# Two attention units side by side ahead of the first FFN tile, weight splits beside the FFN tiles, and the last column two feeds earlier

## What is computed

```python
f = 1.0 / (1.0 + np.exp(-f_logit))
for t in range(S):
    state = f[:, :, t, :, None] * state + np.einsum('bhd,bhe->bhde', k[:, :, t], v[:, :, t])
    y[:, :, t] = np.einsum('bhd,bhde->bhe', q[:, :, t], state)
# x = y by token
h = x @ w_in;  x = where(h > 0, h, exp(min(h, 0)) - 1) @ w_out      # first FFN
h = max(x @ w2_in, 0);  out = (h * h) @ w2_out                      # second FFN
```

## Time and profile before

| | us |
|---|---|
| median of 3 runs | 1048.3 (1048.1, 1048.3, 1054.33) |
| the profiled execution | 1054.74, its span 1052.9 |
| first matmul of the first FFN tile | 100.42 after the span's start |
| attention beside the first FFN | from there to 576.8 |
| FFN alone | from 576.8 to the end |
| PE / DVE / ACT / POOL busy | 982.0 / 537.8 / 384.4 / 292.7 |

### The profile page before, as it was taken

One profiled execution on the slowest core, in us unless ns is written; L12 is line 12 of the kernel. 1 busy time (PEld: TensorE's weight loads), 2 busy tenths in 40 slices (PEclk: granted clock), 3 DMA queues, 4 the chain that ended last, 5 costly groups with the idle time before them and its releaser, 6 DMA issues.

```text
span 1052.9 us, 25949 instructions
## 1 busy us (share of the span) xinstructions
PE 982.0 (93%) x11096; PEld 833.0 (79%) x11096; DVE 537.8 (51%) x769; ACT 384.4 (37%) x694; POOL 292.7 (28%) x240
## 2 busy tenths in 40 slices
PE   7635998899999989999998999999999999999998
PEld 4534787778878868787886887999999999999998
DVE  5753968668566857666442565233233233333322
ACT  1222534444344435344343445233242242322323
POOL 3642636344353525444442365000000000000000
PEclk8655999999999999999999999999999999999999
DMA  6234140221212121211001333001000010000000
GB/s 198 70 118 133 59 117 26 76 74 54 67 60 73 45 76 52 76 58 50 21 17 46 106 98 98 31 1 61 1 31 30 0 60 0 30 30 0 31 1 31
DMA packets 47238, 57.97 MB, mean 55 GB/s; under 512 B 7968, under 2 KB 39456, under 8 KB 47136
## 3 DMA queue, kind: packets, MB, share of 16 engines
q1 hardware_dynamic: 45408, 47.04, 15.0%
q10 hardware_dynamic: 1728, 9.44, 2.4%
HBM read 42.30 MB, written 9.44 MB: 49 GB/s over the span
## 4 chain that ended last, share of the span: by engine, by line
PE 82%; SPq 5%; issue 4%; DVE 4%; DMA 2%; ACT 2%; POOL 1%; DVEq 0%; POOLq 0%; ACTq 0%
PE ps L1192 7%; PE ps L1193 7%; PE ps L1197 7%; PE ps L1231 6%; PE ps L1230 6%; PE ps L1234 6%; PE ps L901 5%; PE ps L903 5%; PE ps L780 5%; PE ps L908 5%; PE ps L922 4%; SPq L258 4%; PE ps L928 4%; PE ps L924 4%; PE ps L827 2%
## 5 line engine op out<-in xcount | busy, mean ns | idle before, releaser
L1146 DVE TENSOR_TENSOR g<-g 128x512 f32<-128x512 f32 x96 | 67.1, 699 | 264.0 <-ACT g L1066 264.0
L485 POOL TENSOR_TENSOR glo<-g,ghi 128x512 fp32r<-128x512 f32 x80 | 109.5, 1369 | 262.9 <-ACT ghi L366 262.9
L1066 ACT ACTIVATE g<-ps 128x512 f32<-128x512 f32 x112 | 67.1, 599 | 286.5 <-PE ps L1197 282.2
L1192 PE MATMUL ps<-xhi,wts 128*128 128x512 f32 x336 | 132.7, 395 | 3.7 <-ACT xhi L351 3.7
L1193 PE MATMUL ps<-xhi,wts 128*128 128x512 f32 x336 | 132.6, 395 | 0.0
L1231 PE MATMUL ps<-wts,ghi 128*128 128x384 f32 x380 | 128.9, 339 | 0.0
L1230 PE MATMUL ps<-wts,ghi 128*128 128x384 f32 x380 | 127.6, 336 | 0.0
L780 PEld LDWEIGHTS ps<-q,k 48*62 48x62 f32 (+6 forms) x4992 | 79.1, 140 | 59.0 <-issue 38.5
L780 PE MATMUL ps<-q,k 48*62 48x32 f32 (+6 forms) x4992 | 85.8, 224 | 39.4 <-DMA q<-qk 10.2
L901 PE MATMUL ps<-xhi,wts 128*128 128x512 f32 x240 | 100.7, 419 | 14.8 <-ACT xhi L351 14.7
L359 ACT ACTIVATE e<-ps 128x512 f32<-128x512 f32 x80 | 47.8, 598 | 176.3 <-PE ps L908 176.2
(11 more groups left out here) (94 smaller groups left out, 1668.2 us busy)
## 6 DMA issues: line engine op xcount, KB each, us to landing
raw<-w SPq DMA_DIRECT2D x64, 192.0 KB, 2.4
gate<-fl SPq DMA_DIRECT2D x12, 512.0 KB, 3.7
q<-qk SPq DMA_DIRECT2D x24, 256.0 KB, 3.8
k<-qk SPq DMA_DIRECT2D x12, 512.0 KB, 3.7
v<-vn SPq DMA_DIRECT2D x12, 384.0 KB, 3.1
x<-xo ACTq DMA_DIRECT2D x6, 768.0 KB, 3.3
xs<-x ACTq DMA_DIRECT2D x6, 768.0 KB, 4.3
out<-PT SPq DMA_DIRECT2D x24, 192.0 KB, 1.9
```

The source lines that it names most:

```text
L485: nc.gpsimd.tensor_tensor(out=glo[:, f % 2, :], in0=g[:, f % 2, :], in1=ghi[:, f % 2, :].bitcast(F32), op=ALU.subtract).then_inc(s_glo, 1)
L1192: nc.tensor.matmul(h, w(0, k), xhi[:, k, :], start=(k == 0), stop=False)
```

## The change

Four things are done.

1. **Units 0 and 1 go through all seven levels side by side.** Unit 1 gets banks of its own (4 and 5, 6 and 7; the accumulators move to banks 4 to 6), and buffers borrowed from tiles of the FFN that are idle then (`e` for its early gate products, `g` for `cross`, `xo` for `krow`, and the first unit's `krow` for its `ys`). Levels alternate between the two pairs of banks. `take` of level 4 is made by ACT for these two units (four instructions of 16 partitions each). The tails follow each other, and only then come the four early levels of unit 2 = (1, 0), with nothing beside them. The warm-up matmuls between the levels are gone, and the scaled queries of level 6 are no longer made for units 0 and 1.
2. **First transfers.** ACT issues the loads of k and the gates of unit 0 and the mask, SP the others; ACT also expands the mask, which DVE did. `v` is doubled and loaded earlier. Half of unit 1's gather is issued by ACT.
3. **Weight splits.** 4 chunks are split ahead of the first tile; the other 28 follow two by two in the tiles f = 0 to 13 of the periods (1, 0) and (1, 1), each behind `activate`, `high` and `low` of its tile.
4. **Last column.** In all later periods it stands behind slot 11 in place of slot 13. ACT's `y_copy` and `last_copy` and DVE's `state_update` move up by one tile.

The diff, cut to its core:

```diff
-PAIR_A, PAIR_Y = 0, 5
-ACC = 2
+PAIR_A, PAIR_Y = 0, 2
+ACC = 4
 HID = 7
-SPLITS = [(2, 2, 2, 2), (2, 2, 2, 2), (3, 3, 2, 2), (2, 2, 1, 1)]
+FIRST_SPLIT = 4
+def split_at(c, f):
+    return [i for i in (2 * f + 4, 2 * f + 5) if c == 1 and i < 2 * NF]
...
+    def pair(c, h, which):
+        if second(c, h):
+            return ps[:, 4:6, :] if which == "A" else ps[:, 6:8, :]
+        return ps[:, PAIR_A:PAIR_A + 2, :] if which == "A" else ps[:, PAIR_Y:PAIR_Y + 2, :]
...
# sync
-        load_gates(0, 0)
         load_q(0, 0)
-        load_k(0, 0)
-        sp.dma_start(mask_words, mask_d).then_inc(s_const, 16)
-        sp.dma_start(ident[:], ident_d).then_inc(s_const, 16)
         load_gates(0, 1)
         load_q(0, 1)
         load_k(0, 1)
+        sp.dma_start(ident[:], ident_d).then_inc(s_const, 16)
         load_v(0, 0)
-        for c in range(NC):
+        load_v(0, 1)
+        load_weights(range(FIRST_SPLIT))
+        load_gates(1, 0)
+        load_gates(1, 1)
+        load_q(1, 0)
+        load_k(1, 0)
+        load_q(1, 1)
+        load_k(1, 1)
+        gather(0, 0)
+        gather(0, 1, range(4))
+        load_weights(range(FIRST_SPLIT, FIRST_SPLIT + 4))
+        load_v(1, 0)
+        for c in range(1, NC):
...
# vector
         for l in range(EARLY):
-            step(0, 0, l, False)
+            for h in range(2):
+                q_update(0, h, l)
+                double(0, h, l)
+            for h in range(2):
+                take(0, h, l)
...
# tensor, in period(c, h)
             values(c, h)
-            feed(c, h, (11, 12, 13))
+            feed(c, h, (11,))
             last_column(c, h)
-            feed(c, h, (14, 15))
+            feed(c, h, (12, 13, 14, 15))
...
# tensor, start
+        for l in range(LEVELS):
+            for h in range(2):
+                product(0, h, l)
+        transpose_keys(0, 0)
+        transpose_keys(0, 1)
+        new_state(0, 0)
+        values(0, 0)
+        new_state(0, 1)
+        last_column(0, 0)
+        values(0, 1)
+        last_column(0, 1)
         for l in range(EARLY):
-            product(0, 0, l)
-            keep_warm(2)
-        for h in range(2):
-            period(0, h)
+            product(1, 0, l)
```

More of the change, by code:

```diff
@@ L174, in products @@
             start = WU - (WU >> (l - 1))
-            return decay_early[:, start:start + (WU >> l)]
+            early = e[:, :, :].rearrange("p i t -> p (i t)") if second(c, h) else decay_early
+            return early[:, start:start + (WU >> l)]
         start = 16 * X - (16 * X >> (l - EARLY))
@@ L189, in nth, with moves @@
         return (c - 1) * NF + f
-    def after(c, h):
-        return (c, h + 1)
+    def moves(c, h, heads):
+        for head in heads:
+            a, j = head // 2, head % 2
+            part = HP * (j ^ (a % 2))
+            at = head * D
+            while at < (head + 1) * D:
+                end = min((head + 1) * D, (at // P + 1) * P)
+                yield (xs[at % P:at % P + end - at, at // P, h % 2 * 2 * C:h % 2 * 2 * C + 2 * C],
+                       ys(c, h)[part + at - head * D:part + end - head * D, a, :])
+                at = end
     def more(c, h, n=1):
@@ L602, in take @@
             else:
-                dve.wait_ge(s_evE, count(c, h, EARLY, l))
-            pair = PAIR_Y if l < EARLY - 1 else PAIR_A
+                dve.wait_ge(*taken(c, h, l))
+            if l < 2 and not past(c, h, 2):
+                dve.wait_ge(s_mask, 2)
+                dve.wait_ge(s_zero, 2)
             w = 1 << l
```

467 lines of the change are left out of this document (258 added, 209 removed).

## The result

The changed kernel takes 1005.77 us (median of four runs, 1003.77 to 1008.18), the one before 1051.32 beside it (1048.1 to 1054.63). The ratio is 0.9568, 95% interval 0.9519 to 0.9616: 45.5 us less. The forecast was 1011. The profiled execution took 1007.56 us, its span is 1005.6, so 47.2 less than that of before, where the prediction's sum had 40.5.

What follows compares the result with a forecast made beforehand. Latency between PE, DVE and POOL was taken to bound the first stage, PE the rest. Terms: -26.4 - 10.5 - 2.6 - 6 + 5 = -40.5, profile 1014; median between 1013.8 and 1007.8, forecast 1011, range 995 to 1028.

Steps and rivals of the forecast that it cites:

- Inputs and levels: First stage: unit 1's last operand lands at 14 us, and seven levels of two units end at 44.4 us.
- The contention term: Levels of units 0 and 1: DVE and POOL delaying each other adds 3 us to the path.
- the rival: First stage: DVE and POOL take turns throughout, 3 us become 14, first tile at 83 to 86, total 1022; chance 0.15.
- Tails: First stage: transposes 3.8 us, then one unit's tail at half clock, 5.4, and one at full, 3.1, ending at 56.7.
- Unit 2's levels and the two products ahead of the tile: End of first stage: four uncovered levels, 15.4 us, and two more products, 1.9, put the first tile at 74.
- Splits: Chunk 1's tiles: 28 splits in place of 16 cost +5 us, 2.5 for each of two periods.
- Last column and gather: Chunk starts: earlier last column removes waits for xhi, -10.5 and -2.6 us, and half clock behind them, -6.
- the one estimated: Behind the gaps at chunk starts: lost clock recovered, 1.7 us at chunk 3's start, -6 us for three starts together.
- DVE as chunk 1's bound: Chunk 1: each of 14 tiles with a split loses 0.9 us, 12.6 in place of 5, total 1019; chance 0.18.
- Gaps that stay: Chunk starts: last column waits for state_update, gather starts as late as before, 1011 + 19 = 1030; chance 0.07.
- PE at half clock all through: Chunk 1: waits in every tile hold PE at half clock, +85 us, total 1096; chance 0.02.
- Better: Tail and unit 2 at full clock, first tile at 68, and splits hidden: total 1000; chance 0.15.

Runs made afterwards that it cites:

- all splits in the best order: The later splits and the double ahead, with DVE's splits of slots 2 to 4 moved one place later still: 992.90 us, ratio 0.9452.
- part 4 alone: Only the earlier last column, with y_copy, last_copy and state_update one tile up, put into the kernel before: 1025.86 us, ratio 0.9792.
- tiny splits: Changed kernel with DVE's and POOL's low splits of 28 chunks cut to 8 columns, same order: 995.22 us, ratio 0.9480.
- the run with PE kept busy: Changed kernel plus two idle matmuls behind each of unit 2's early products: 1007.44 us; with the later splits and the double ahead too, 1000.24.
- the double ahead: Changed kernel with DVE's double ahead of q_update in the side-by-side levels: 1004.95 us; with the later splits too, 997.45 us.
- the later splits: Changed kernel with two splits of DVE and one of POOL moved behind the level work that stood behind them: 1000.18 us, ratio 0.9525.
- the edit: The later splits and the double ahead, with unit 3's q and k loads issued behind the gather: 998.31 us, ratio 0.9506.

## Why the prediction was right, and where it wasn't

**The stages and their signs** were all as forecast, and the sizes within 2 us for the first two. The bound was read rightly: a shorter start and the gaps, and nothing else. Nearly all of what is gained lies there. That the first stage came within 1.8 us of the forecast is in part luck: its levels were 4.3 us too long and its last piece 3.1 too short, as the next paragraphs show, and two executions of the kernel before differ by 3.8 us in this stage. It was also read as bound by latency between PE, DVE and POOL; the 7.13 us behind a weight load and the two waits for `q` were part of it and were left out.

**Inputs and levels.** Forecast: levels end at 44.4. Measured: PE's last product ends at 40.15. The four levels with `take` on DVE ended at 33.7 (forecast 32.2). The three late ones were 3.1 us each, not 3.75: the term had `k_update` at 1.36 us, and it took 1.05 to 1.16. The contention term was 3 us; the excess of DVE's operations over their length alone is 8.4 us in sum (doubles 1.52 to 1.99 for the wide ones, 1.01 to 1.12 for the small ones, two query updates of 1.5). It did not lengthen the path by that much: much of it passed while DVE would have waited for a product that itself waited for POOL.

**The rule weighed.** Of the excess the prediction had 3 us and the rival 14; measured are 8.4. A `double` takes 0.21 us for 64 columns with POOL idle and 1.02 for 16 beside its key update, and it ends when that ends (38.35 and 38.33 us); turning the order exchanged 4.2 us of DVE for 2.1 of POOL. The Trainium skill (SBUF — State Buffer, "SBUF: two separate sides") says that two such instructions exclude each other for the whole instruction, and the trace agrees. What failed is the price of the rival that was built on it, 14 us on the path. By these rows, taking turns costs the path only where both have work that the next product waits for.

**Tails.** Forecast 12.3 us from transposes to unit 2's first product, measured 11.7 with a pause of 2.49 in it that was not foreseen, so 9.2 of work. I had put one unit at half clock and one at full; `new_state` takes 0.93 us for both, near the 0.85 of full clock, so both ran at full and only the start of the transposes did not. Two errors, 3.1 too long and 2.5 not foreseen, nearly cancelled.

**Unit 2's levels and the two products ahead of the tile.** Forecast 17.3, measured 20.4: the piece was mis-sized by 3.1 us. The levels were right: from 51.76 to 68.75 us they take 17.0, of which 1.68 are the second pause, so 15.3 against 15.4. Their price already had the products near half clock, and they ran there (1.93, 1.82, 1.72 us). What failed is the pause, not foreseen, and the term of 1.9 us for the last two products, which is full clock: they took 3.4 at a granted clock of 0.50.

**Gather and `xhi`.** `xhi` was ready at 63.4, forecast 67, and nothing waited for it.

**Splits.** +6.8 against +5, with the cause as forecast: an early slot's split waits for ACT's, and the levels queue behind it. The size was put at 2.5 us for a period; the longest wait ahead of level 3 went from 1.56 to 3.07 and 3.09, and half clock stands behind each: 7.4 us of clock lost from 72 to 178 (2.3 of it behind the first tile, 5.1 behind the two waits), against 3.9 from 100 to 200 before. The prediction named DVE's queue; POOL's had its split in front of the same levels. The experiments show more than the prediction saw. The order was not good before either: 98.5 us without the gap, against 93.1 with all splits in the best order. And part 4 alone brought chunk 1's stretch to 94.4 us with the 16 splits of before, 4.1 less than its gap explains. Beside that, the new splits cost 10.9, not 6.8: the step compared with a stretch that another part of the change would have shortened. In the trace with part 4 alone PE is idle for 2.7 us less than before, the gap left out (the wait ahead of level 3 in the second period is 0.49 in place of 1.56, one of 0.70 and one of 0.51 are gone, one of 0.94 is 0.56) and its busy time is 1.4 less: the half clock that stood behind the first wait of 1.56 is missing, with a wait of the same length. Why part 4 does this, and only without the new splits (107.9 less its gap of 2.9 is 105.0, against 105.3), stays open, and these are single traces.

**Last column and gather.** -25.8 against -19.1, the largest miss. The gaps went as forecast: the starts of chunks 2 to 5 had 10.5 us together and have none, and of the last 3.7 there is 0.69 left, not 1.1: -13.5 in all. A term that was mis-sized is the one estimated, -6 for the clock behind the gaps. Clock lost from 200 us to the end was 8.5 us before (5.1 behind the starts of the chunks, 3.4 from 574 to 582 behind the last) and is nil. That is 2.5 of the miss of 6.7. Some 4 us remain, which the prediction had no term for: from chunk 2 on, PE before had four more pauses of 0.21 to 0.52 us in `values` and one wait of 0.56 for a key update, 2.3 in all. These went too, for a reason that I did not test.

**The median.** The gain is 45.5 us by medians and 47.2 by profiles, 1.7 apart. The prediction had allowed for up to 6 between the two and taken half of it off. That caution (3.2 us) and the 6.7 us of the paragraph before, less these 1.7 and less the 3.0 by which the kernel before was slower this time, are the 5.2 us that 1011 is too high; the errors of the two stages ahead of it, -1.8 and +1.8, cancel, which is luck. The prediction took the 6.4 us between the runs of before for half clock; the 3.8 us found in the first stage suggest that a part of it is something else.

**The rivals.** DVE as chunk 1's bound at +12.6 did not come; but by the stretch with tiny splits, 12.2 us of chunk 1 do hang on them. Gaps that stay, and PE at half clock all through, did not come either. "Better" asked for unit 2's levels at full clock and hidden splits: the first brings no more than it costs, as the run with PE kept busy shows, and the second can be had entirely.

## What to carry to other kernels

A short wait of PE can have a second price, the half clock behind it: waits of 3.07 and 3.09 us both had it here, of those of 1.56 us one had it and another not, those of 1.33 had none. Ask for the granted clock behind each gap, not only for its length, before the gap is priced. Work that is moved beside the tiles is paid by its place in an in-order queue: look for what stands behind an instruction that itself waits for another engine, and put that first; here a few such moves gave 12 us in one stretch and took no work away. When two engines exclude each other, an order that frees the one loads the other, so only the operation that the next product waits for is worth protecting.

## What the hardware showed that was not expected

**The granted clock at the start of a trace can be wrong.** The first product of 64 matmuls took 1.93 us in the changed kernel, where the recorded clock is 1.00, and 1.12 us in the kernel with the double ahead, whose recorded clock falls to 0.50 only behind it. From 12 to 42 us the first says 1.00 and the second 0.50, yet the products are equally long (3.64 and 3.63 us for level 0 and 1). At 43 us both run `new_state` at full clock or near it (0.93 and 1.12 us), and from there on both records show the falls that the durations show. It is the same in all eleven traces of this family of kernels: in the seven whose first product takes 1.93 us the record is 1.00 until it falls between 49 and 53 us, in the four in which it takes 1.12 it falls between 8 and 10 us. The reading that fits them all is that the record holds changes only, so that an execution that begins at half clock shows 1.00 until it has risen and fallen once. So the 0.86 of the first stage above is too high, and a duration is the better witness: 1.9 us for 64 such products is half clock, 1.03 to 1.12 full.

**Transfers can stop PE without a wait.** A pause of 2.39 us (2.49 in the changed kernel, 3.79 with the later splits) fell to 0.57 when the 351 GB/s ahead of it became 27, and one of 1.02 us appeared where the moved loads ran. Another one of 1.68 us in the changed kernel, inside unit 2's first product, is not explained by this: it was 1.01 without and 1.24 with the edit.

**A fifth of a microsecond of work can take one.** A `double` of 16 columns took 1.02 us beside POOL, while one of 64 took 0.21 when POOL was idle; in chunk 1 it is the same (94.41 us above, 8 columns, 1.01 us), and with the later splits, where POOL is idle at that point, this one takes 0.16.
